# First layer of a fused attention and two-layer kernel in tiles of 256 and 384 tokens, and a shorter start

## The chip, the cores and the metric

The kernel runs on one core of a Trainium2 chip. The metric is the device time of one execution in microseconds. A core has five engines with an instruction queue each: TensorE (PE, matmuls; its weight loads are shown as PEld), VectorE (DVE), ScalarE (ACT), GpSimd (POOL) and SyncE (SP), which here only issues DMAs. They work on SBUF, and matmuls write the banks of PSUM; semaphores order them.

## The reference

Windowed attention over 4 x 576 tokens with 8 heads of 64, then two dense blocks on the 2304 x 512 result.

```python
# q, k, v: (4, 8, 576, 64)
rel = pos[:, None] - pos[None, :]
mask = (rel >= 0) & (rel < 64)
scores = np.where(mask, np.matmul(q, k.T) / 8, -1e9)      # k.T: last two axes
attn = np.exp(scores - scores.max(-1)); attn /= attn.sum(-1) + 1e-09
x = attn @ v                                   # to (2304, 512)
h = x @ moe_w_in;   g = s * max(h, 0)**2 + b;               x = g @ moe_w_out
h = x @ moe2_w_in;  g = max(h, 0) + alpha * min(h, 0);      out = g @ moe2_w_out
# w_in: (512, 2048), w_out: (2048, 512), s and b scalars, alpha: (2048,)
```

## The kernel before, in words

Every operand of the dense layers is split into a high part (rounded to fp32r) and a low part (the rest), and each product is three matmuls: high by high, high by low, low by high.

**Attention** goes in 18 groups of 128 tokens (`j`). For a group TensorE computes the scores (`scores`, L313, 64x128 blocks), VectorE adds the mask and takes the maxima (`maxima`, L498 to L507), ScalarE the exponents (`exponents`, L392, in two halves of four), VectorE divides by the sum (`normalise`, L518), TensorE transposes (L322), both copy (`copy_pt`, L400 and L524), TensorE multiplies by v (`values`, L334), and ScalarE and VectorE write the result as high and low part into `x` (`x_high` L406, `x_low` L530).

**A dense layer** is cut into tiles of 384 tokens, six per layer, and each tile into 16 steps, one for each 128 columns of the hidden width. Step `c` has an `up(c)`: 12 matmuls of 384 columns into the PSUM bank `hid[c % 2]` (L252), and a `down(c)` in two halves: in the first layer 12 matmuls of 384 columns into four accumulators `acc` (L291), in the second 9 of 512 columns into three (L297). Between them stands the chain of the step. First layer: relu on ScalarE (L367), times itself and s on VectorE (L474), high part with b added on ScalarE (L377), low part on VectorE (L488). Second layer: L479, L482, L380, L492.

**The order is written out by hand**, engine by engine, as one loop over steps. TensorE does `down(c)`, then `up(c + 2)`, so `up` is two steps ahead. In a step `s` ScalarE does relu and high part of `c = s + 1`, then what the attention has for it in this step (`copy_pt`, `x_high`), two weight splits in tile 0, and the exponents; VectorE does square and low part of `s + 1`, `copy_pt`, `x_low`, `normalise`, `maxima`. Behind all that, in the last step of a tile, both copy the accumulators out (`copy_out`, L426 and L548). The attention of the next tile's groups runs beside a tile: `group_at` gives the slot of a group, slots 5 steps apart, the first in the last step of the tile before; scores in step `slot`, the exponents' halves in `slot` and `slot + 1`, `normalise` in `slot + 2`, transposes in the middle of `down(slot + 3)`, values in the middle of `down(slot + 4)`.

**The start.** Groups 0, 1 and 2 are computed ahead of the loop; after each, `first_ups` does the part of `up(0)` and `up(1)` on its 128 tokens. Then come `scores(3)` and `up(2)`.

**Weights** arrive in pieces of 256 KB, four slots in SBUF, w_in and w_out in turn. GpSimd makes high and low part of the first 8 pieces; for the others ScalarE makes the high part (L387) and GpSimd the low part (L246), two pieces per step of tile 0. The second layer's are split in the first layer's last tile. The first layer's result goes through DRAM (`x2_scratch`) and comes back tile by tile.

Of the kernel before, what the change touches and what calls it, by code (L numbers as in the profile page):

```python
# [15 lines left out]
def build(nc, qk_in, v_in, w_in_a, w_out_a, w_in_b, w_out_b, consts_in, out):  # L16
# [6 lines left out]
    TILE = 384  # L23
    NO = TILE // 128
    NT = TOKENS // TILE
# [6 lines left out]
    assert TOKENS % TILE == 0 and NT % 2 == 0 and ND == PAIRS  # L32
# [6 lines left out]
    arrives = {piece: n + 1 for n, piece in enumerate(PIECES)}  # L39

    def slot_of(j):
        return NF * (j // NO - 1) + PITCH * (j % NO) - 1

    group_at = {slot_of(j): j for j in range(NO, NJ)}

    with ExitStack() as ctx:
# [8 lines left out]
        x = sb("x", [128, 2, 2, ND, TILE], F32R)  # L55
        g = sb("g", [128, 2, 2, TILE], F32R)
        relu = sb("relu", [128, 2, TILE])
        outs = sb("outs", [128, ND * TILE])
# [3 lines left out]
        x2_in = qk[:, 0:ND * TILE].rearrange("p (c t) -> p c t", c=ND)  # L62
# [19 lines left out]
        x2_dram = nc.dram_tensor("x2_scratch", (NT, 128, ND * TILE), F32, kind="Internal").ap()  # L82
# [12 lines left out]
        w_split = sem("w_split")  # L95
# [12 lines left out]
        last_copied = [sem(f"last_copied{a}") for a in range(NO)]  # L108
# [17 lines left out]
        def banks(j):  # L126

            return ((bank_x, bank_y), (acc[0], acc[1]), (acc[2], acc[3]))[j] if j < NO else (bank_x, bank_y)

        def x_at(j):  # L130
            return j // NO % 2, slice(j % NO * 128, (j % NO + 1) * 128)

# [9 lines left out]
        def _(sp):  # L142
            def load_piece(n):
                down, f = PIECES[n % NP]
                if n % NP >= SLOTS or n >= NP:
                    sp.wait_ge(w_split, n - SLOTS + 1)
                src = ((w_in_a, w_out_a), (w_in_b, w_out_b))[n // NP][down][f]
                sp.dma_start(piece[:, n % SLOTS, :], src).then_inc(piece_here[n // NP][n % SLOTS], 16)
# [11 lines left out]
            def store(dst, src, t):  # L160
                sp.wait_ge(acc_read_act, t + 1)
                sp.wait_ge(acc_read_dve, t + 1)
                sp.dma_start(dst, src).then_inc(stored, 16)

            def load_x2(t):
                sp.dma_start(qk[:, 0:ND * TILE], x2_dram[t - NT]).then_inc(x2_loaded, 16)

            load_qk(0)
            load_qk(1)
            load_v(0)  # L170
            load_piece(0)
# [8 lines left out]
            load_v(2)  # L180
            load_piece(6)
            load_piece(7)
            load_qk(3)
            for n in range(8, BY_POOL + SLOTS):
                load_piece(n)
            load_v(3)
            load_qk(4)
            load_v(4)
            for i in range(NF):
                for n in range(BY_POOL + SLOTS + 2 * i, min(BY_POOL + SLOTS + 2 * i + 2, NP)):  # L190
                    load_piece(n)
                if i == 1:
                    load_qk(5)
                if i == 5:
                    load_v(5)
                    load_qk(6)
            load_v(6)
            load_qk(7)
            load_v(7)
            for t in range(1, NT - 1):  # L200
                store(x2_dram[t - 1], outs[:, :], t - 1)
                for j in range(NO * t + 5, min(NO * t + 8, NJ)):
# [4 lines left out]
            store(x2_dram[NT - 2], outs[:, :], NT - 2)  # L207
            sp.wait_ge(s_done, NJ)
            sp.wait_ge(stored, 16)
            load_x2(NT)  # L210
            for n in range(NP + SLOTS, 2 * NP):
                load_piece(n)
            store(x2_dram[NT - 1], outs[:, :], NT - 1)
            out_v = out.rearrange("(t a p) d -> t p a d", p=128, a=NO)
            for t in range(NT, 2 * NT - 1):
                sp.wait_ge(x2_lo, ND * (t - NT + 1))
                sp.wait_ge(stored, 16 * (t - NT + 2))
                load_x2(t + 1)
                store(out_v[t - NT], outs[:, 0:NO * DM].rearrange("p (a d) -> p a d", a=NO), t)
            for a in range(NO):  # L220
# [442 lines left out]
```

## Time and profile before

| | |
|---|---|
| median of three runs | 910.15 us (909.05 to 910.41) |
| the profiled execution | 910.64 us, span 908.9 us |
| granted TensorE clock | 1.0 |
| TensorE busy, matmuls | 886.0 us (97%) |
| VectorE busy | 410.2 us (45%) |
| ScalarE busy | 285.9 us (31%) |
| GpSimd busy | 91.5 us (10%) |

All rows come from the profiled execution, whose own time is 1.7 us over its span. Busy times are sums over instructions; an engine can be busy 45% on average and still be late in one stage. In rows of the timeline the instructions of one line that follow on each other are merged, and the end of a matmul contains its way through the array, so the time of a block of matmuls is read from its start to the start of the next.

### The profile page before, as it was taken

How to read it: one execution, taken by the hardware profiler on the slowest of the kernel's cores; microseconds unless marked ns; L12 is line 12 of the kernel's file. 1: busy time of each engine (PE TensorE's matmuls, PEld its weight loads, DVE VectorE, ACT ScalarE, POOL GpSimd, SP SyncE). 2: the span in 40 equal slices, each digit the busy share in tenths (PEclk: the TensorE clock that was granted, in tenths of full speed). 3: DMA queues.
4: the chain of work that ended last, by engine and by line, in shares of the span. 5: the costliest groups of instructions: out<-in, count | busy, mean ns of one | idle time of the engine just before them, and what ended most of it. 6: DMA issues, size and time to landing. Idle time of an engine off the chain costs nothing.

```text
span 908.9 us, 13847 instructions
## 1 busy us (share of the span) xinstructions
PE 886.0 (97%) x5664; PEld 831.9 (92%) x5664; DVE 410.2 (45%) x945; ACT 285.9 (31%) x717; POOL 91.5 (10%) x81
## 2 busy tenths in 40 slices
PE   4799999999999999999999999999999999999998
PEld 4799999999999999999999999999999999999987
DVE  5155544444444444444354444454453444444443
ACT  4156543434434443444455211111121111111111
POOL 5135500000000000000356200000000000000000
PEclk9999999999999999999999999999999999999999
DMA  6425421102112110300344200200200200200000
GB/s 232 167 79 166 123 87 54 53 25 78 39 53 88 53 53 24 129 6 1 122 124 127 93 0 1 70 1 1 70 1 1 70 0 1 70 1 1 35 1 35
DMA packets 18767, 53.06 MB, mean 58 GB/s; under 512 B 2064, under 2 KB 2064, under 8 KB 18704
## 3 DMA queue, kind: packets, MB, share of 16 engines
q1 hardware_dynamic: 18704, 52.18, 17.5%
q8 instruction: 44, 0.72, 0.3%
q14 instruction: 19, 0.16, 0.1%
HBM read 42.74 MB, written 9.44 MB: 57 GB/s over the span
## 4 chain that ended last, share of the span: by engine, by line
PE 91%; ACT 4%; DVE 3%; DMA 1%; issue 1%; DVEq 0%
PE hid L252 44%; PE acc L297 22%; PE acc L291 20%; PE bank_x L334 2%; ACT p L392 2%; PE bank_x L313 1%; DMA qk<-in_qk 1%; PE bank_x L322 1%; PE bank_y L322 1%; DVE relu L474 1%; ACT g L377 1%; DVE g L488 1%; DVE p L518 1%; ACT relu L367 1%; PE acc L322 0%
## 5 line engine op out<-in xcount | busy, mean ns | idle before, releaser
L252 PE MATMUL hid<-x,w_in 128*128 128x384 f32 (+1 forms) x2352 | 447.8, 340 | 4.5 <-DVE x L530 4.5
L252 PEld LDWEIGHTS hid<-x,w_in 128*128 128x128 f32 x2352 | 418.1, 193 | 16.1 <-DVE x L530 5.1
L291 PE MATMUL acc<-g,w_out 128*128 128x384 f32 x1152 | 223.6, 337 | 2.7 <-ACT outs L426 2.7
L297 PE MATMUL acc<-w_out,g 128*128 128x512 f32 x864 | 215.4, 393 | 0.4 <-DVE g L492 0.4
L291 PEld LDWEIGHTS acc<-g,w_out 128*128 128x128 f32 x1152 | 199.8, 188 | 4.8 <-issue 3.8
L297 PEld LDWEIGHTS acc<-w_out,g 128*128 128x128 f32 x864 | 160.7, 188 | 30.0 <-DVE g L492 0.8
L380 ACT ACTIVATE g<-relu 128x384 fp32r<-128x384 f32 x96 | 50.4, 525 | 332.7 <-DVE relu L482 332.7
L474 DVE SCALAR_TENSOR_TENSOR relu<-relu,consts 128x384 f32<-128x384 f32 x96 | 71.0, 739 | 165.6 <-ACT relu L367 165.6
L479 DVE TENSOR_SCALAR relu<-hid,consts 128x384 f32<-128x384 f32 x96 | 59.3, 617 | 161.5 <-PE hid L252 161.5
L488 DVE SCALAR_TENSOR_TENSOR g<-relu,consts,g 128x384 fp32r<-128x384 f32 x96 | 59.9, 624 | 65.8 <-ACT g L377 65.8
L367 ACT ACTIVATE relu<-hid 128x384 f32<-128x384 f32 x96 | 46.8, 488 | 132.6 <-PE hid L252 132.6
L377 ACT ACTIVATE g<-relu,consts 128x384 fp32r<-128x384 f32 x96 | 59.2, 617 | 78.7 <-DVE relu L474 78.7
L492 DVE TENSOR_TENSOR g<-relu,g 128x384 fp32r<-128x384 f32 x96 | 53.6, 559 | 56.8 <-ACT g L380 56.8
L246 POOL TENSOR_TENSOR w_in<-piece,w_in 128x512 fp32r<-128x512 f32 x32 | 43.8, 1371 | 330.9 <-ACT w_in L387 330.5
L392 ACT ACTIVATE p<-p,negmx 128x128 f32<-128x128 f32 x144 | 56.0, 390 | 42.0 <-DVE negmx L507 42.0
L482 DVE SCALAR_TENSOR_TENSOR relu<-hid,relu 128x384 f32<-128x384 f32 x96 | 53.5, 557 | 3.3
L246 POOL TENSOR_TENSOR w_out<-piece,w_out 128x512 fp32r<-128x512 f32 x32 | 42.5, 1332 | 73.8 <-ACT w_out L387 73.5
L392 ACT ACTIVATION_READ_ACCUMULATOR p<-p,negmx 128x1 f32 x144 | 27.0, 187 | 0.0
L518 DVE TENSOR_TENSOR p<-p,rowrec 128x1024 f32<-128x1024 f32 x18 | 25.0, 1390 | 0.6
L313 PE MATMUL bank_x<-qk 64*64 64x128 f32 x256 | 19.3, 294 | 4.8 <-DMA qk<-in_qk 4.8
L507 DVE CUSTOM_DVE_ANT_0 p<-bank_x,mask 128x128 f32<-128x128 f32 x64 | 18.3, 286 | 11.7 <-DVE mask L498 6.5
L313 PEld LDWEIGHTS bank_x<-qk 64*64 64x64 f32 x256 | 15.2, 143 | 8.4 <-issue 8.3
(54 smaller groups left out, 314.6 us busy)
## 6 DMA issues: line engine op xcount, KB each, us to landing
qk<-in_qk SPq DMA_DIRECT2D x18, 640.0 KB, 5.0
v<-in_v SPq DMA_DIRECT2D x18, 512.0 KB, 3.6
x_scratch<-outs SPq DMA_DIRECT2D x6, 768.0 KB, 4.0
qk<-x_scratch SPq DMA_DIRECT2D x6, 768.0 KB, 5.7
piece<-in_w_in_a SPq DMA_DIRECT2D x16, 256.0 KB, 2.8
piece<-in_w_out_a SPq DMA_DIRECT2D x16, 256.0 KB, 3.0
piece<-in_w_in_b SPq DMA_DIRECT2D x16, 256.0 KB, 2.8
piece<-in_w_out_b SPq DMA_DIRECT2D x16, 256.0 KB, 2.6
```

What stands on the lines that cost most here:

```text
L246: pool.tensor_tensor(lo, piece[:, n % SLOTS, :], hi.bitcast(F32), ALU.subtract).then_inc(w_split, 1)
L252: mm = pe.matmul(hid[f % 2][:, at], w_in[:, wi, f, dc, :], x[:, par, xi, dc, at], start=(dc == 0 and n == 0), stop=(dc == ND - 1 and n == 2))
L291: mm = pe.matmul(acc[dc][:, 0:TILE], w_out[:, wi, f, dc * 128:(dc + 1) * 128], g[:, f % 2, gi, :], start=(f == 0 and n == 0), stop=(f == N ...
L297: mm = pe.matmul(acc[a][:, :], g[:, f % 2, gi, a * 128:(a + 1) * 128], w_out[:, wi, f, :], start=(f == 0 and n == 0), stop=(f == NF - 1 an ...
L367: act.activation(relu[:, c % 2, :], hid[c % 2][:, 0:TILE], ACT.Relu).then_inc(hid_read, 1)
L377: act.activation(g[:, c % 2, 0, :], relu[:, c % 2, :], ACT.Identity, bias=b_sb).then_inc(g_hi, 1)
L392: act.activation(p[:, j % 2, i, :], p[:, j % 2, i, :], ACT.Exp, bias=negmx[:, j % 2, i:i + 1], scale=-1.0, accum_out=rowsum[:, j % 2, i:i ...
L474: dve.scalar_tensor_tensor(out=relu[:, c % 2, :], in0=relu[:, c % 2, :], scalar=s_sb, in1=relu[:, c % 2, :], op0=ALU.mult, op1=ALU.mult).t ...
L479: dve.tensor_scalar(relu[:, c % 2, :], hid[c % 2][:, 0:TILE], 0.0, alpha[:, f:f + 1], ALU.min, ALU.mult).then_inc(negative, 1)
L482: dve.scalar_tensor_tensor(out=relu[:, c % 2, :], in0=hid[c % 2][:, 0:TILE], scalar=0.0, in1=relu[:, c % 2, :], op0=ALU.max, op1=ALU.add). ...
L488: dve.scalar_tensor_tensor(out=g[:, c % 2, 1, :], in0=relu[:, c % 2, :], scalar=b_sb, in1=g[:, c % 2, 0, :].bitcast(F32), op0=ALU.add, op1 ...
L492: dve.tensor_tensor(g[:, c % 2, 1, :], relu[:, c % 2, :], g[:, c % 2, 0, :].bitcast(F32), ALU.subtract).then_inc(g_ready, 1)
```

## The change

- The first layer has seven tiles instead of six: three of 256 tokens, then four of 384. The second keeps its six of 384. `widths` and `starts` hold this; `C_A` is the number of steps of the first layer (112), `C_END` that of all (208).
- Only groups 0 and 1 are computed ahead of the loop, and `first_ups` is gone: after them come `scores(2)` and whole `up(0)`, `up(1)`, `up(2)` of 256 columns. Groups 2 and 3 run beside tile 0, 4 and 5 beside tile 1, 6 to 8 beside tile 2, then three per tile.
- The low parts of the first layer's w_out pieces from piece 8 on are made by VectorE (`split_low`), those of w_in by GpSimd. `w_split` becomes two semaphores.
- `copy_out` stands right behind relu and high part, or square and low part, ahead of the attention work of the step; ScalarE copies banks 0 and 2, VectorE 1 and 3 (in the second layer 1), each copy signals on its own, and TensorE waits bank by bank (`acc_free`).
- SyncE's order of loads in the start is another; the scratch tensor is laid out by 128 columns of d_model, so rows of 1 KB or 1.5 KB are written and rows of 1.5 KB read, where they were 6 KB.

```diff
+    WIDE = 384
+    NB = WIDE // 128
+    widths = [256] * 3 + [WIDE] * ((TOKENS - 768) // WIDE) + [WIDE] * (TOKENS // WIDE)
+    starts = [sum(widths[:t]) % TOKENS for t in range(len(widths))]
+    NT = len(widths)
+    NA = NT - TOKENS // WIDE
+    C_A, C_END = NA * NF, NT * NF
+    EARLY = widths[0] // 128
...
+    def by_dve(n):
+        return BY_POOL <= n < NP and PIECES[n][0] == 1
...
     def slot_of(j):
-        return NF * (j // NO - 1) + PITCH * (j % NO) - 1
+        t = tile_of(j)
+        return NF * (t - 1) + PITCH * (j - starts[t] // 128) - 1
...
             load_qk(0)
             load_qk(1)
+            load_piece(0)
             load_v(0)
-            load_piece(0)
             load_piece(1)
             load_v(1)
             sp.dma_start(consts[:, :], consts_in).then_inc(consts_here, 16)
-            load_qk(2)
             load_piece(2)
             load_piece(3)
+            load_qk(2)
...
-            for j in range(NO):
+            for j in range(EARLY):
                 scores(j)
-            for j in range(NO):
+            for j in range(EARLY):
                 transposed(j)
                 values(j)
-                first_ups(j)
-            scores(NO)
-            up(LAG)
-            for c in range(2 * NT * NF):
+            scores(EARLY)
+            for c in range(LAG + 1):
+                up(c)
+            for c in range(C_END):
...
+            def acc_free(t, n):
+                if n % 2 == 0:
+                    pe.wait_ge(acc_read_act, 2 * (t - 1) + n // 2 + 1)
+                elif t <= NA:
+                    pe.wait_ge(acc_read_dve, 2 * (t - 1) + n // 2 + 1)
+                else:
+                    pe.wait_ge(acc_read_dve, 2 * NA + t - NA)
...
                     hi(c)
+                if i == NF - 1 and t >= 0:
+                    copy_out(t)
                 if s - 3 in group_at:
                     copy_pt(group_at[s - 3])
...
-                if i == NF - 1 and t >= 0:
-                    copy_out(t)
...
+            def split_low(n):
+                high, low = weights(n)
+                dve.wait_ge(piece_hi, n - BY_POOL + 1)
+                dve.tensor_tensor(low, piece[:, n % SLOTS, :], high.bitcast(F32),
+                                  ALU.subtract).then_inc(split_dve, 1)
...
+                if t == 0:
+                    for n in range(BY_POOL + 2 * i, min(BY_POOL + 2 * i + 2, NP)):
+                        if by_dve(n):
+                            split_low(n)
                 if s - 2 in group_at:
                     normalise(group_at[s - 2])
```

The rows below are the instructions in program order: line, operation, output and inputs, shape and count. On TensorE, the start before, from the scores of groups 1 and 2 to those of group 3 (L313 scores, L322 transposes, L334 values, L252 the parts of `up(0)` and `up(1)`):

```order
L313 MATMUL acc<-qk 64x128 x32
L322 MATMUL bank_x<-ident,p 128x128 x4
L322 MATMUL bank_y<-ident,p 128x128 x4
L334 MATMUL bank_x<-pt,v 64x64 x16
L252 MATMUL hid<-x,w_in 128x128 x24
L322 MATMUL acc<-ident,p 128x128 x8
L334 MATMUL acc<-pt,v 64x64 x16
L252 MATMUL hid<-x,w_in 128x128 x24
L322 MATMUL acc<-ident,p 128x128 x8
L334 MATMUL acc<-pt,v 64x64 x16
L252 MATMUL hid<-x,w_in 128x128 x24
L313 MATMUL bank_x<-qk 64x128
```

And now (L346 scores, L355 transposes, L367 values, L295 `up`, L320 `down`):

```order
L346 MATMUL acc<-qk 64x128 x16
L355 MATMUL bank_x<-ident,p 128x128 x4
L355 MATMUL bank_y<-ident,p 128x128 x4
L367 MATMUL bank_x<-pt,v 64x64 x16
L355 MATMUL acc<-ident,p 128x128 x8
L367 MATMUL acc<-pt,v 64x64 x16
L346 MATMUL bank_x<-qk 64x128
L346 MATMUL bank_y<-qk 64x128
...
L295 MATMUL hid<-x,w_in 128x256 x36
L320 MATMUL acc<-g,w_out 128x256 x24
```

One group's transposes and values and all 128-column matmuls on `hid` have left the start; 36 matmuls of 256 columns stand between `scores(2)` and the first `down`.

On VectorE, two steps of tile 0 with a group's second maxima (the last of them shown) and its `normalise`, before:

```order
L507 ISA p,negmx<-bank_y,mask 128x128
L507 ISA negmx 128x1
L474 SCALAR_TENSOR_TENSOR relu<-relu,consts 128x384
L488 SCALAR_TENSOR_TENSOR g<-relu,consts,g 128x384
L513 TENSOR_SCALAR rowsum<-rowsum 128x8
L515 RECIPROCAL rowrec<-rowsum 128x8
L518 TENSOR_TENSOR p<-p,rowrec 128x1024
```

And now:

```order
L539 ISA p,negmx<-bank_y,mask 128x128
L539 ISA negmx 128x1
L499 SCALAR_TENSOR_TENSOR relu<-relu,consts 128x256
L514 SCALAR_TENSOR_TENSOR g<-relu,consts,g 128x256
L524 TENSOR_TENSOR w_out<-piece,w_out 128x512
L545 TENSOR_SCALAR rowsum<-rowsum 128x8
L547 RECIPROCAL rowrec<-rowsum 128x8
L550 TENSOR_TENSOR p<-p,rowrec 128x1024
```

The low part of a w_out piece (L524) stands between the step's low part and `normalise`.

On ScalarE, the end of a tile whose last step has a group's scores (L367 relu, L377 high part, L392 exponents, L426 accumulators), before:

```order
L367 ACTIVATE relu<-hid 128x384
L377 ACTIVATE g<-relu,consts 128x384
L392 ACTIVATE p,rowsum<-p,negmx 128x128 x4
L426 ACTIVATE outs<-acc 128x384 x2
L367 ACTIVATE relu<-hid 128x384
```

And now:

```order
L401 ACTIVATE relu<-hid 128x256
L409 ACTIVATE g<-relu,consts 128x256
L455 ACTIVATE outs<-acc 128x256 x2
L424 ACTIVATE p,rowsum<-p,negmx 128x128 x4
L401 ACTIVATE relu<-hid 128x256
```

The two copies moved ahead of the exponents.

## Rows read from the trace of the kernel before

**Rows 1.** Waits of TensorE: line, released by, us in total, times, longest.

```profile
PE acc L313 <- DMA qk<-in_qk: 4.4, 1, 4.4
...
PE acc L291 <- ACT outs L426: 2.7, 4, 0.7
...
PE bank_x L322 <- DVE p L518: 0.3, 2, 0.2
```

**Rows 2.** Timeline of the start: start, duration (us), engine, line, operation; idle before.

```profile
11.28 1.97 DVE L518 TENSOR_TENSOR p<-p,rowrec 128x1024 f32<-128x1024 f32 x1
...
37.80 1.93 PE L322 MATMUL acc<-ident,p 128*128 128x128 f32 x8
...
39.76 0.60 ACT L400 ACTIVATE pt<-acc 128x512 f32<-128x512 f32 x1 [8.18 <-PE acc L322]
...
43.99 5.38 PE L252 MATMUL hid<-x,w_in 128*128 128x128 f32 x24 [1.41 <-DVE x L530]
...
51.22 4.11 PE L252 MATMUL hid<-x,w_in 128*128 128x384 f32 x12
55.16 4.33 PE L291 MATMUL acc<-g,w_out 128*128 128x384 f32 x24
```

**Rows 3.** TensorE at pace: timeline, and busy times by stretch (131.50:209.27 is one tile).

```profile
125.28 2.25 PE L291 MATMUL acc<-g,w_out 128*128 128x384 f32 x12
128.49 2.35 PE L252 MATMUL hid<-x,w_in 128*128 128x384 f32 x12
...
509.20 2.27 PE L252 MATMUL hid<-x,w_in 128*128 128x384 f32 x12
...
511.30 2.24 PE L297 MATMUL acc<-w_out,g 128*128 128x512 f32 x9
...
513.38 2.27 PE L252 MATMUL hid<-x,w_in 128*128 128x384 f32 x12
...
131.50:209.27 77.77, 77.10 (x600) 74.49 (x601) 34.93 (x103) 31.66 (x89) 0.00 (x0) 1.00 0.17 57
```

**Rows 4.** Timeline, ScalarE and VectorE: the chain of one step behind `up`.

```profile
121.31 0.49 ACT L367 ACTIVATE relu<-hid 128x384 f32<-128x384 f32 x1 [2.71 <-PE hid L252]
...
121.84 0.62 DVE L474 SCALAR_TENSOR_TENSOR relu<-relu,consts 128x384 f32<-128x384 f32 x1 [2.51 <-ACT relu L367]
...
122.49 0.62 ACT L377 ACTIVATE g<-relu,consts 128x384 fp32r<-128x384 f32 x1 [0.69 <-DVE relu L474]
...
123.14 0.62 DVE L488 SCALAR_TENSOR_TENSOR g<-relu,consts,g 128x384 fp32r<-128x384 f32 x1 [0.69 <-ACT g L377]
```

**Rows 5.** Timeline, ScalarE and VectorE: the steps of one group, at a tile's end.

```profile
128.96 0.40 ACT L392 ACTIVATE p<-p,negmx 128x128 f32<-128x128 f32 x1 [1.69 <-DVE negmx L507]
...
130.52 0.84 ACT L426 ACTIVATE outs<-acc 128x384 f32<-128x384 f32 x2
131.26 0.47 ACT L367 ACTIVATE relu<-hid 128x384 f32<-128x384 f32 x1
...
133.94 0.40 ACT L392 ACTIVATE p<-p,negmx 128x128 f32<-128x128 f32 x1 [0.89 <-DVE negmx L507]
...
135.94 0.49 ACT L367 ACTIVATE relu<-hid 128x384 f32<-128x384 f32 x1 [0.35 <-PE hid L252]
...
138.74 1.23 DVE L518 TENSOR_TENSOR p<-p,rowrec 128x1024 f32<-128x1024 f32 x1
```

**Rows 6.** Groups by line and shape, VectorE's copies: busy us, mean ns of one.

```profile
L548 DVE COPY outs<-acc 128x384 f32<-128x384 f32 x12 | 6.1, 549 | 0.0
...
L550 DVE COPY outs<-acc 128x512 f32<-128x512 f32 x5 | 3.4, 685 | 0.1
```

**Rows 7.** Timeline of tile 0: ScalarE's splits of a step, and a square on VectorE.

```profile
54.92 0.62 ACT L387 ACTIVATE w_out<-piece 128x512 fp32r<-128x512 f32 x1
...
55.97 0.39 ACT L392 ACTIVATE p<-p,negmx 128x128 f32<-128x128 f32 x1
...
62.17 1.63 DVE L474 SCALAR_TENSOR_TENSOR relu<-relu,consts 128x384 f32<-128x384 f32 x1
```

More of the change, by code:

```diff
@@ L38, in build, with tile_of @@
     NP = len(PIECES)
-    arrives = {piece: n + 1 for n, piece in enumerate(PIECES)}
+    place = {piece: n for n, piece in enumerate(PIECES)}
+    def by_dve(n):
+        return BY_POOL <= n < NP and PIECES[n][0] == 1
+    def tile_of(j):
+        return next(t for t in range(NA) if starts[t] <= j * 128 < starts[t] + widths[t])
     def slot_of(j):
-        return NF * (j // NO - 1) + PITCH * (j % NO) - 1
-    group_at = {slot_of(j): j for j in range(NO, NJ)}
+        t = tile_of(j)
+        return NF * (t - 1) + PITCH * (j - starts[t] // 128) - 1
+    group_at = {slot_of(j): j for j in range(EARLY, NJ)}
     with ExitStack() as ctx:
@@ L126, in banks, with split_count @@
         def banks(j):
-            return ((bank_x, bank_y), (acc[0], acc[1]), (acc[2], acc[3]))[j] if j < NO else (bank_x, bank_y)
+            return ((bank_x, bank_y), (acc[0], acc[1]))[j] if j < EARLY else (bank_x, bank_y)
         def x_at(j):
-            return j // NO % 2, slice(j % NO * 128, (j % NO + 1) * 128)
+            t = tile_of(j)
+            return t % 2, slice(j * 128 - starts[t], (j + 1) * 128 - starts[t])
+        def split_count(n):
+            same = sum(by_dve(m) == by_dve(n) for m in range(n + 1))
+            return (split_dve if by_dve(n) else split_pool), same
         block = ctx.enter_context(nc.Block())
@@ L192, in _ @@
                 if i == 1:
+                    load_qk(4)
+                if i == 4:
+                    load_v(4)
+                if i == 5:
                     load_qk(5)
-                if i == 5:
+                if i == 9:
                     load_v(5)
[L196 to L202, printed above, removed]
+            for t in range(1, NA - 1):
+                store(t - 1)
+                for j in range((starts[t + 1] + 256) // 128, min((starts[t + 1] + widths[t + 1] + 256) // 128, NJ)):
                     load_qk(j)
@@ L274, in up @@
+                if c >= 2:
+                    pe.wait_ge(hid_read, c - 1)
+                if t in (0, NA):
+                    pe.wait_ge(*split_count(NP * (t // NA) + place[0, f]))
+                if f == 0 and t < NA:
+                    pe.wait_ge(x_lo, (starts[t] + n_tok) // 128)
+                if f == 0 and t >= NA:
+                    pe.wait_ge(x2_lo, ND * (t - NA + 1))
                 for dc in range(ND):
-                    mm = up_part(t % 2, f, dc, slice(0, TILE))
+                    for n, (wi, xi) in enumerate(((0, 0), (0, 1), (1, 0))):
+                        mm = pe.matmul(hid[f % 2][:, 0:n_tok], w_in[:, wi, f, dc, :], x[:, t % 2, xi, dc, 0:n_tok],
+                                       start=(dc == 0 and n == 0), stop=(dc == ND - 1 and n == 2))
```

250 lines of the change are left out of this document (114 added, 136 removed).

## The prediction

> **What bounds the kernel now.** I read the waits of TensorE first. Outside the start it waits for almost nothing: the largest entry that belongs to the loop is 2.7 us in four waits for ScalarE's copy of the accumulators [rows 1]. So the loop runs at the pace of the matmuls, and only three things can move the time: when the loop starts, how many matmul nanoseconds it holds, and whether the other engines still keep up once a step is shorter.
>
> The timeline of the start shows the first. The first `down` begins at 55.16 [rows 2]. Ahead of it stand three groups' attention and three runs of 24 matmuls with 128 columns, each 5.38 us long, at about 220 ns a matmul; even after the last of them, which began at 43.99, the 12 matmuls of 384 columns that start at 51.22 take 3.94 us, 328 ns each. Only from 55.16 on are they at 174 to 180 ns (4.33 us for 24). The granted clock of the page is 1.0 in every slice, so that row doesn't show it; the durations say that TensorE ran at 1.2 GHz until 55.16 and at 2.4 GHz behind it; before it rose it had done 5.3 us of 128-column matmuls, scores, and 3.94 us of 384-column ones.
>
> The second comes from the steady state: 12 matmuls of 384 columns take 2.10 us (509.20 to 511.30; 2.08 in the first layer, 173.6 ns each), 9 of 512 take 2.08 (231 ns) [rows 3]. A tile of the first layer takes 77.77 us; 16 steps of 24 matmuls are 66.7 of it and one accumulator wait 0.7 [rows 1], which leaves 10.4, or **3.5 us per attention group**. Scores cost 3.21 - 2.08 = 1.13 us.
>
> The third is the chain behind each `up`: relu, square, high part, low part start 0.53, 0.65 and 0.65 us apart and the last takes 0.62 [rows 4]. It is done 2.65 us after the matmuls of `up` ended, and TensorE needs the result only two blocks, 4.17 us, later: 1.5 us to spare. In the steps of a group the exponents stand in ScalarE's queue, 1.56 us for a half (128.96 to 130.52) [rows 5]. The relu behind the second half still waited 0.35 us for TensorE, so it was just not late.
>
> **The change, term by term.** Times are of the profiled execution, 910.64 us (span 908.9), 0.5 above the median of 910.15.
>
> *Start.* The product p of group 0 is normalised at 13.25 [rows 2]; nothing waits for a third group's queries any more (the 4.4 us in [rows 1]), so its transposes start at 13.3. ScalarE copies them 1.96 later (39.76 against 37.80), at 15.3, then does the last half of group 1's exponents until 17.4. Normalising group 1 meets GpSimd's weight splits and takes 0.4 + 1.97: transposes of group 1 at 19.8. From transposes to the first matmul on x it is 6.19 us (37.80 to 43.99): 26.0. There `scores(2)` stands first, because it waits for x_lo of both groups, 1.95 us at half clock; `up(0)` at 27.9. 12 matmuls of 256 columns at half clock take 2.7 us; if the clock rises 3.94 us into them, as before, 18 are at half clock and 18 at 117.5 ns (below): **`down(0)` at 34.0 instead of 55.16: -21.1 us**. If the clock comes 3 us sooner or later, this moves by 1.5.
>
> *Matmuls of the loop.* Behind that point the first three tiles have 48 + 45 blocks of 12 instead of 32 + 29. A matmul of 256 columns isn't in the trace. From below: the line through 512 and 384 gives 114.6 ns, and the 128-column runs at half clock, halved, say that a weight load allows 108 to 112. From above: 384's cost less 128/2.4 is 120.3 (all of its surplus fixed), and 173.6 if the load of new weights set the pace of the 384-column stream. I take 117.5, between the two near rows. 93 x 12 x 0.1175 = 131.1 against 61 x 12 x 0.1736 = 127.1: **+4.0 us** (+0.8 to +7.2 between the near ends). The Trainium skill (TensorE: Matmul & The Clock Gate, Back-to-back issue gap) gives N/2.4 + 2.5 ns, an estimate of 109.2 here; for 384 columns it gives 162.5 where the trace has 173.6, so the trace doesn't agree. By that rule for both widths this term would be 2.9 us.
>
> *One more group in the loop* (group 2's transposes and values, group 3's scores): **+3.5 us**, from the same row as above.
>
> *Steps of 256 columns, tiles 1 and 2.* Copies lose 136 ns per 128 columns on VectorE [rows 6], ScalarE about 0.11; so relu to square is 0.42, then 0.52, 0.54, and low part 0.49. I lay one group out from the end of `up(s+1)`, a block being 1.41 us. `down(s)` to 1.41, scores to 2.54, exponents start 0.47 behind (128.49 to 128.96), at 3.01, and end at 4.57. Relu(s+2) at 4.57, its low part starts at 6.05. The second half's exponents start 0.87 behind the low part's start now (131.26 to 133.94 less 1.81), 0.74 with the narrower one: 6.79 to 8.35. Relu(s+3) is queued behind them, at 8.35 instead of 7.07. Its low part is ready at 10.35, and `down(s+3)`, due at 9.69, waits 0.7. The multiplication of `normalise` is queued behind that low part: it starts 0.97 behind its start now (135.94 to 138.74 less 1.83), 0.84 then, takes 1.23 and ends at 11.9; the transposes, half a block behind 10.4, i.e. at 11.1, wait 0.85. **1.55 us per group**, where groups in tiles of 384 have none. Groups 4 and 6 are scored at a tile's end, where VectorE now copies two banks before `maxima`: exponents 0.7 later, 2.25 each. Three at 1.55 and two at 2.25 make **+9.2 us**. A faster or slower matmul changes only the part of the five steps that isn't set by this chain, about half.
>
> *Tile 0.* ScalarE has two splits per step besides, 1.05 us (54.92 to 55.97 in [rows 7]); VectorE gets one low part of a w_out piece, about 0.6, right ahead of `normalise` and `maxima`; GpSimd keeps one of 1.3 us. Where an operation of VectorE with both inputs in SBUF falls on one of GpSimd's, it ends behind it: the square at 62.17 took 1.63 instead of 0.62, a normalisation 1.97 instead of 1.23. Laid out the same way, group 3 costs 1.5 (relu(s+3) at 9.3) and 2.2 (normalised at 14.2, transposes due at 12.0): 3.7. Group 2, whose exponents stand between relu(0) and relu(1) while TensorE already has three `up` behind it, costs 1.65 + 1.7 + 2.25 = 5.6. In plain steps ScalarE's own round (relu, wait for a square held up by GpSimd, high part, two splits) is 3.3 us against TensorE's 2.82: 0.5 in each of three steps. Sum 10.8; before, late normalisations made TensorE wait 0.3 [rows 1]. **+10.5 us**, 7 to 14. The rule of the Trainium skill on that port (SBUF — State Buffer, Who interferes with whom) is that whoever starts first holds it for the whole instruction and the other blocks fully; the trace agrees (0.62 against 1.63), and the rule speaks against giving VectorE a share of the splits, though GpSimd's share halves.
>
> *Accumulators.* The four waits go, **-2.7 us**: the copy of a bank now starts when `down` ends, and with 256 columns 0.4 us each hides behind `up`'s 1.4. The stores and x2 loads with shorter rows, and the other order of the weight and query loads, I count at nothing: a x2 load has over half a tile before its first use, and pieces are asked for two steps (6.6 us) ahead of their use. If the queries and values that stand between them in SyncE's queue hold them up, tile 0 gets 1 to 4 us longer; that is in its upper end.
>
> Sum: -21.1 + 4.0 + 3.5 + 9.2 + 10.5 - 2.7 = **+3.4 us**, span 912.3, 914.0 in a profiled execution, 913.5 against the median.
>
> **Rivals.**
> *Faster: the short steps hide their chains.* It decides at one place: the relu behind the second half of the exponents. If the chain of 256 columns is 0.7 us shorter than I make it, or exponents start earlier, relu(s+3) is in time, `down(s+3)` doesn't wait and the normalisation comes in time too. For it: before, the same place was met with 0.35 to spare, so two engines' overheads have been small. Against: the exponents (1.56 us a half) don't shrink with the tile, the steps do, by 1.35 us each. With half of the 20 us of waits gone the time is 903.5; with all gone 894.
> *Worse tile 0.* Pieces late, or TensorE, idle half the time in group 2's steps, back at 1.2 GHz for some microseconds: +4 to +8, 918 to 922. For it: four slots of pieces now turn over in 6.6 us instead of 8.3; against: in tile 0 before, the waits of TensorE name no piece [rows 1].
> *Weight loads set the pace at 256 columns.* With 145 ns a matmul, about +16 to +30 us, 930 to 943. Against: with the same load the 128-column runs took about 220 ns at half clock [rows 2], so 110 at full clock if the load goes with it.
>
> **How the numbers follow.** Forecast 55 (own range 909 to 918, of which 14 within the bound below), faster rival 27 (6 of it within), worse tile 0 12, weight loads 6. A measurement of this kernel tells 0.2%, 1.8 us, from no change: faster than 908.3, 0.21; within 0.20; slower than 912.0, 0.59. Range 904 to 921: it leaves out the deep end of the faster rival (8 in 100), the weight loads, and the far end of tile 0.
>
> **What would show it.** Right: `down(0)` near 34; 12 matmuls of 256 columns every 1.41 us; in each group of tiles 1 and 2 TensorE waits for g and then for p, 0.7 to 0.85 us each; tile 0 takes about 63 us from `down(0)` to tile 1, of which 11 are waits; tiles of 384 columns keep 77.1. The `acc` waits gone. Wrong: `up` blocks of over 1.5 us, no waits for g or p in tiles 1 and 2, or ScalarE waiting for pieces.

## The result, and the profile after

The change makes the kernel about 1% slower. The median is 918.94 us (918.77 to 920.44, 4 runs), against 910.25 for the kernel before on the same chip: a ratio of 1.0102 [1.0085, 1.012]. Forecast were 913.5, in a range of 904 to 921. The profiled execution took 918.83 (span 917.0) where the one before took 910.64 (span 908.9): +8.1 us of span to be explained, where the sum gave +3.4.

The waits of TensorE in the profile after (line, released by, us in total, times, longest):

```profile
PE bank_x L355 <- DVE p L550: 12.2, 8, 4.4
PE acc L320 <- DVE g L514: 8.3, 9, 2.5
PE bank_x L346 <- DMA qk<-in_qk: 4.8, 1, 4.8
```

Of [rows 1] the waits for ScalarE's copy of the accumulators are gone, as forecast. New are 8.3 us for g and 12.2 for p; 4.4 of the latter is the start's first group. So the kernel traded a late start for a loop in which VectorE's results are late. Cut into stretches, the span shows where (start:end, length, then the busy time of PE, PEld, DVE, ACT and POOL, the granted clock, the DMA share, GB/s). The stretches are from the first `down` to tile 1, tile 1, tile 2, the first layer's four wide tiles, and two pieces of tile 0:

```profile
33.08:100.27 67.19, 56.87 (x519) 54.44 (x517) 40.26 (x102) 35.93 (x97) 14.29 (x11) 0.92 0.37 115
100.27:156.62 56.35, 53.98 (x531) 51.95 (x530) 25.56 (x81) 23.41 (x71) 0.00 (x0) 1.00 0.16 53
156.62:219.35 62.73, 59.08 (x602) 56.14 (x601) 30.55 (x105) 27.88 (x89) 0.00 (x0) 1.00 0.20 67
219.35:515.20 295.85, 295.85 (x2153) 289.24 (x2153) 134.20 (x338) 130.38 (x331) 39.32 (x31) 1.00 0.22 69
37.20:39.92 2.72, 2.72 (x12) 2.72 (x13) 1.51 (x9) 2.27 (x10) 1.29 (x1) 0.50 0.29 96
68.70:74.30 5.60, 5.60 (x26) 5.60 (x27) 2.21 (x4) 2.14 (x4) 1.28 (x1) 0.50 0.22 57
```

And of the kernel before, its tile 0 and its last four tiles of the first layer, between the same events:

```profile
55.16:131.50 76.34, 75.35 (x589) 72.18 (x589) 42.81 (x102) 41.89 (x111) 33.39 (x24) 1.00 0.38 116
209.27:507.10 297.83, 296.50 (x2152) 289.36 (x2153) 134.42 (x338) 129.46 (x325) 40.77 (x32) 1.00 0.22 70
```

From these the ledger of the span: the first `down` starts at 33.08 instead of 55.16 [rows 2], -22.1. The first 768 tokens take 67.19 + 56.35 + 62.73 = 186.3 us instead of 76.34 + 77.77 = 154.1 [rows 3], +32.2. The four wide tiles take 2.0 less. The second layer takes 401.8 in both. Together +8.1. The columns say more than the lengths: in the wide tiles PE is busy for the whole stretch, in tile 0 for 56.87 of 67.19 us, and there the granted clock is 0.92, with two pieces at 0.50. The two pieces are the work that follows a wait in this part of TensorE's timeline (start, duration, line, operation; idle before):

```profile
27.71 5.53 PE L295 MATMUL hid<-x,w_in 128*128 128x256 f32 x36
...
33.08 1.61 PE L320 MATMUL acc<-g,w_out 128*128 128x256 f32 x12
37.20 2.93 PE L320 MATMUL acc<-g,w_out 128*128 128x256 f32 x12 [2.50 <-DVE g L514]
39.92 1.69 PE L295 MATMUL hid<-x,w_in 128*128 128x256 f32 x12
...
45.11 0.65 PE L355 MATMUL bank_x<-ident,p 128*128 128x128 f32 x4 [2.42 <-DVE p L550]
...
60.78 1.70 PE L320 MATMUL acc<-g,w_out 128*128 128x256 f32 x12 [1.30 <-DVE g L514]
...
65.31 0.98 PE L320 MATMUL acc<-g,w_out 128*128 128x256 f32 x6 [1.39 <-DVE g L514]
68.70 1.12 PE L355 MATMUL bank_x<-ident,p 128*128 128x128 f32 x4 [2.41 <-DVE p L550]
...
71.75 2.71 PE L295 MATMUL hid<-x,w_in 128*128 128x256 f32 x12
```

Rows of twelve matmuls that read 1.6 us at full clock read 2.71 and 2.93 after the waits of 2.50 us and of 1.30 + 1.39 + 2.41 us: TensorE is at 1.2 GHz there (granted clock 0.50). The wait of 2.42 alone at 45.11 was not followed by a slow stretch.

What is late in tile 0 stands in VectorE's and GpSimd's rows ahead of the transposes at 45.11:

```profile
41.18 0.48 DVE L514 SCALAR_TENSOR_TENSOR g<-relu,consts,g 128x256 fp32r<-128x256 f32 x1 [0.64 <-ACT g L409]
...
41.70 0.69 DVE L524 TENSOR_TENSOR w_out<-piece,w_out 128x512 fp32r<-128x512 f32 x1
...
42.27 1.26 POOL L278 TENSOR_TENSOR w_in<-piece,w_in 128x512 fp32r<-128x512 f32 x1 [3.24 <-ACT w_in L419]
42.31 1.25 DVE L545 TENSOR_SCALAR rowsum<-rowsum 128x8 f32<-128x8 f32 x1
...
43.83 1.22 DVE L550 TENSOR_TENSOR p<-p,rowrec 128x1024 f32<-128x1024 f32 x1
```

VectorE does its share of the weight splits (L524), during which GpSimd begins its own, and the tiny operation on 8 row sums that should follow takes 1.25 us; it ends with GpSimd's. The same operation takes 0.17 elsewhere (below). So the multiplication of `normalise` begins 2.2 us after the end of g's low part at 41.66, not 0.4. By the rule that the prediction weighed (Trainium skill, SBUF — State Buffer, Who interferes with whom), whoever issues first gets the ports that VectorE and GpSimd share for its whole instruction, and the other is blocked. The trace agrees, here even for an operation on 8 elements a partition (1.25 against 0.17).

### The profile page after: what moved, and what is told of

Same layout as the page of the kernel before. It is cut to its first block, busy times and chain, and to the rows that moved or that the text cites. A ratio compares the mean times of both kernels' runs of the same rounds, so it can differ in the third digit from the quotient of the medians.

```text
span 917.0 us, 14625 instructions
## 1 busy us (share of the span) xinstructions
PE 882.8 (96%) x6000; PEld 828.6 (90%) x6000; DVE 421.1 (46%) x992; ACT 293.4 (32%) x751; POOL 73.8 (8%) x68
## 4 chain that ended last, share of the span: by engine, by line
PE 87%; DVE 6%; ACT 5%; issue 1%; POOL 0%; DVEq 0%; ACTq 0%; POOLq 0%
PE hid L295 41%; PE acc L330 22%; PE acc L320 19%; ACT p L424 3%; PE bank_x L367 2%; DVE relu L499 1%; DVE p L550 1%; PE bank_x L346 1%; ACT g L409 1%; PE bank_x L355 1%; PE bank_y L355 1%; DVE g L514 1%; ACT relu L401 1%; DVE p L539 1%; DVE rowsum L545 0%
## 5 line engine op out<-in xcount | busy, mean ns | idle before, releaser
L295 PE MATMUL hid<-x,w_in 128*128 128x384 f32 (+1 forms) x2496 | 441.3, 325 | 0.0
L295 PEld LDWEIGHTS hid<-x,w_in 128*128 128x128 f32 x2496 | 412.8, 190 | 11.2 <-issue 2.9
L320 PE MATMUL acc<-g,w_out 128*128 128x384 f32 (+1 forms) x1344 | 231.8, 317 | 8.5 <-DVE g L514 8.3
L320 PEld LDWEIGHTS acc<-g,w_out 128*128 128x128 f32 x1344 | 208.3, 191 | 12.0 <-DVE g L514 10.9
L499 DVE SCALAR_TENSOR_TENSOR relu<-relu,consts 128x384 f32<-128x384 f32 (+1 forms) x112 | 71.5, 639 | 164.9 <-ACT relu L401 164.7
L514 DVE SCALAR_TENSOR_TENSOR g<-relu,consts,g 128x384 fp32r<-128x384 f32 (+1 forms) x112 | 63.3, 565 | 78.1 <-ACT g L409 78.1
L409 ACT ACTIVATE g<-relu,consts 128x384 fp32r<-128x384 f32 (+1 forms) x112 | 63.9, 571 | 99.6 <-DVE relu L499 95.3
L401 ACT ACTIVATE relu<-hid 128x384 f32<-128x384 f32 (+1 forms) x112 | 49.2, 439 | 125.9 <-PE hid L295 125.9
L278 POOL TENSOR_TENSOR w_out<-piece,w_out 128x512 fp32r<-128x512 f32 x19 | 25.6, 1348 | 24.8 <-ACT w_out L419 24.6
L346 PE MATMUL bank_x<-qk 64*64 64x128 f32 x272 | 20.4, 292 | 6.3 <-DMA qk<-in_qk 4.8
L346 PEld LDWEIGHTS bank_x<-qk 64*64 64x64 f32 x272 | 16.0, 143 | 9.4 <-issue 8.5
L355 PE MATMUL bank_x<-ident,p 128*128 128x128 f32 x68 | 11.6, 296 | 12.2 <-DVE p L550 12.2
```

Of the source, the lines that this page charges most:

```text
L278: pool.tensor_tensor(lo, piece[:, n % SLOTS, :], hi.bitcast(F32), ALU.subtract).then_inc(split_pool, 1)
L295: mm = pe.matmul(hid[f % 2][:, 0:n_tok], w_in[:, wi, f, dc, :], x[:, t % 2, xi, dc, 0:n_tok], start=(dc == 0 and n == 0), stop=(dc == ND - ...
L320: mm = pe.matmul(acc[dc][:, 0:n_tok], w_out[:, wi, f, dc * 128:(dc + 1) * 128], g[:, f % 2, gi, 0:n_tok], start=(f == 0 and n == 0), stop= ...
L401: act.activation(relu[:, c % 2, at], hid[c % 2][:, at], ACT.Relu).then_inc(hid_read, 1)
L409: act.activation(g[:, c % 2, 0, at], relu[:, c % 2, at], ACT.Identity, bias=b_sb).then_inc(g_hi, 1)
L499: dve.scalar_tensor_tensor(out=relu[:, c % 2, at], in0=relu[:, c % 2, at], scalar=s_sb, in1=relu[:, c % 2, at], op0=ALU.mult, op1=ALU.mult ...
```

## The experiments

All ratios are against the kernel before, timed on the same chip in the same rounds.

**1. The accumulators alone.** The kernel before, with the copies bank by bank, ahead of the attention work, and a wait for each bank:

```diff
-                act.wait_ge(down_done, (t + 1) * NF)
-                for n in range(2):
-                    ins = act.activation(outs[...], acc[n][:, 0:width], ACT.Copy)
-                ins.then_inc(acc_read_act, 1)
+                for n in (0, 2):
+                    act.wait_ge(down_done, (t + 1) * NF)
+                    act.activation(outs[...], acc[n][:, 0:width], ACT.Copy).then_inc(acc_read_act, 1)
...
+                        if f == 0 and t > 0:
+                            acc_free(t, dc)
```

> The kernel before with one part of the change alone: accumulators copied bank by bank ahead of the attention work, ScalarE banks 0 and 2, VectorE 1 and 3, TensorE waiting bank by bank. Theory (the four waits of TensorE for outs, 2.7 us, go and nothing comes in their place in tiles of 384): 2.4 to 2.8 us less than before, span 906.3. Rival (the copies now push the exponents back, and the relu behind them is late, 0.35 us was its margin): two waits for g at each tile's end, time within 1 us of before.

Measured: 906.41 us, 0.9963 [0.995, 0.9976], span 904.6. No wait names the copies any more. From the first `down` to the end the kernel is 2.9 us shorter, so this part of the change is worth its 2.7 us. The other 1.4 of the 4.3 us of span lies at the start, where the first `down` begins at 53.77 although nothing was changed there: 0.5 before the 12 matmuls of 384 columns (50.72 instead of 51.22), and 0.9 in them, which took 3.05 us instead of 3.94, because TensorE reached 2.4 GHz within them. The granted clock, which reads 1.0 throughout the start in the profile before, shows the rise in this one:

```profile
50.72 3.21 PE L252 MATMUL hid<-x,w_in 128*128 128x384 f32 x12
53.77 4.32 PE L297 MATMUL acc<-g,w_out 128*128 128x384 f32 x24
```

```profile
50.00:52.00 2.00, 2.00 (x20) 1.67 (x13) 0.93 (x9) 0.81 (x5) 0.00 (x0) 0.50 0.00 0
52.00:54.00 2.00, 2.00 (x12) 2.00 (x11) 0.62 (x1) 1.31 (x7) 0.00 (x0) 0.85 0.03 8
54.00:56.00 2.00, 2.00 (x13) 2.00 (x12) 1.45 (x9) 2.00 (x6) 0.88 (x1) 1.00 0.00 0
```

**2. Everything but the narrow tiles.** The kernel after with 384 tokens in every tile and three groups alone, whole `up`s kept:

```diff
-    widths = [256] * 3 + [WIDE] * ((TOKENS - 768) // WIDE) + [WIDE] * (TOKENS // WIDE)
+    widths = [WIDE] * (2 * TOKENS // WIDE)
```

> The changed kernel with tiles of 384 in both layers and three groups ahead of the loop, then scores(3) and whole up(0), up(1), up(2) of 384 columns; copies and splits as in the changed kernel. It asks what of the start's gain came from the parts of 128 columns and what from the third group, and what the narrow tiles cost. Theory: the parts of 128 columns at half clock (3 x 5.4 us) were most of the long start and can go without narrow tiles; down(0) starts near 40 to 42 instead of 55.2, the loop is as before less the 2.7 us of accumulator waits, span 891 to 895, that is 15 to 18 us under before and 23 to 26 under the changed kernel. Rival (the gain of the start needs the group to go as well; with three groups the attention chains of the start are the bound): down(0) later than 48, span above 900.

Measured: 908.13 us, 0.9982 [0.9972, 0.9991], span 906.4. The size was missed by more than 11 us: the first `down` came at 44.81 (10.3 earlier than before, as whole `up`s of 384 columns replace three runs of 128), but from the first `down` to the end it took 861.6 us instead of 853.7, which gave most of that back:

```profile
PE bank_x L355 <- DVE p L554: 5.4, 3, 2.0
...
PE acc L320 <- DVE g L518: 1.6, 2, 1.1
```

So even wide tiles wait for p here, and 50:60 and 81:93 ran at a granted clock of 0.88 and 0.86. What stands ahead of p in this loop, and didn't in the one before, is VectorE's share of the splits. Experiments 4 and 6 take it out.

**3. Shorter exponents.** The kernel after with one exponent instruction over four heads in each half of groups 2 to 8, with the maximum and the sum of one head, which leaves out part of the computation:

```diff
-                for i in range(4 * half, 4 * half + 4):
-                    act.wait_ge(max_done, HEADS * j + i + 1)
+                    act.wait_ge(max_done, HEADS * j + 4 * half + 4)
+                    ph = p[:, j % 2, 4 * half:4 * half + 4, :]
+                    act.activation(ph, ph, ACT.Exp, ...).then_inc(exp_done, 4)
```

> The changed kernel, but for groups 2 to 8 (those beside tiles of 256 tokens) the four exponents of a half are one instruction over 512 columns with one head's maximum and sum, so a half takes about 0.6 us of ScalarE instead of 1.56; this leaves out part of the computation. Theory (the waits in narrow tiles come from the exponents' time in ScalarE's queue, which doesn't shrink with the tile): relu(s+3) is in time; the waits for g (8.3 us) and for p in tiles 1 and 2 (3.0) nearly vanish, the ones in tile 0 halve; 8 to 12 us less than the changed kernel, span 905 to 909. Rival (VectorE's normalise, queued behind the low part, and its clash with GpSimd make the waits): the waits for p stay at 0.6 in tiles 1 and 2 and 2.4 in tile 0, less than 4 us gained.

Measured: 919.08 us, 1.0098 [1.0079, 1.0118]. The waits for p stay at 0.60 and 2.42 and nothing is gained, as the rival had it. Yet the test doesn't decide, for it hardly shortened what it was to shorten: the one instruction must wait for all four maxima, three of them 0.21 us apart behind the first, and takes 0.72 itself, so the half ended only about 0.2 us sooner than with four exponents (1.56). Experiment 7 puts the question again.

**4. All splits on GpSimd.**

```diff
-        return BY_POOL <= n < NP and PIECES[n][0] == 1
+        return False
```

> The changed kernel with all low parts of the weights on GpSimd again, none on VectorE. Theory (GpSimd's operations hold back VectorE's, so two of 1.3 us in a step of 2.88 us hurt more than VectorE's own 0.6): tile 0 gets 2 to 6 us longer, by squares of over 1 us in plain steps. Rival (the low part right ahead of maxima and normalise is what makes tile 0's waits long): tile 0 gets 1 to 3 us shorter.

Measured: 913.61 us, 1.0043 [1.0028, 1.0058], span 911.9: 5.1 us shorter than the kernel after. The theory that VectorE's share helps GpSimd keep up, and so pays, is refuted; the rival holds, with more than the 1 to 3 us that it was given. In tile 0 the two waits for p fall from 2.42 and 2.41 to 1.31 and 1.47. The operations that GpSimd holds up are still there, as before (a normalisation of 2.10 us, a square of 1.50), but VectorE does less in between. Both slow stretches are still there too: the clock is 0.50 in 37.27:40 and again behind the wait of 1.47 (64.77:67).

**5. TensorE kept awake.** 64 matmuls of 256 columns into the unread half of a bank, ahead of five waits of tile 0; nothing reads what they add:

```diff
+            def filler(n):
+                for _ in range(n):
+                    pe.matmul(acc[1][:, 256:512], w_in[:, 0, 0, 0, :], x[:, 0, 0, 0, 0:256], start=False, stop=False)
...
+    FILL_G = {1: 16, 6: 8, 7: 8}
+    FILL_T = {2: 16, 3: 16}
```

> The changed kernel with 64 extra matmuls of 256 columns that nothing reads, in columns 256 to 511 of an accumulator bank, in tile 0 ahead of its five long waits: 16 ahead of down(1), 8 each ahead of down(6) and down(7), 16 ahead of each of the transposes of groups 2 and 3. They take 1 to 1.9 us each and end before what TensorE waits for. Theory (TensorE falls to 1.2 GHz behind its idle stretches; of the two half-clock stretches of the changed kernel, 37.2 to 39.9 is covered by a wait of the same length, 68.7 to 74.3 is paid): no stretch at clock 0.5 in tile 0 behind 33, 2 to 3 us less, span 914 to 915. Rival (the chain of ScalarE and VectorE sets the time there too): within 1 us of the changed kernel, waits longer by what the matmuls get faster.

Measured: 916.75 us, 1.0071 [1.0056, 1.0086], span 915.0: 2.0 us less than after. The clock of tile 0 is now 1.00:

```profile
33.46:99.00 65.54, 61.57 (x589) 59.14 (x588) 40.56 (x103) 36.74 (x101) 14.37 (x11) 1.00 0.41 123
```

So the fall to 1.2 GHz costs the kernel after about 2 us net. In part the faster matmuls only wait again: ahead of the third `down` there is now a wait for g of 1.39 us that the kernel after doesn't have.

```profile
42.11 0.98 PE L329 MATMUL acc<-g,w_out 128*128 128x256 f32 x6 [1.39 <-DVE g L525]
```

**6. Wide tiles, all splits on GpSimd.** Experiment 2 with the edit of experiment 4.

> The kernel with three groups alone, whole ups and tiles of 384, now with all low parts of the weights on GpSimd as before. Theory (VectorE's split right ahead of normalise, and the row sums held up behind it by GpSimd, made the waits of 5.4 us for p and 1.6 us for g in tile 0): these shrink to the 0.2 to 0.9 us of the kernel before, and the half-clock stretches behind them go too: 5 to 7 us less, span 899 to 902, about 8 us under before. Rival (they come from the shorter start, in which pieces and exponents are late): at most 2 us less, waits for p over 3 us.

Measured: 899.03 us, 0.9881 [0.9864, 0.9897], span 897.1: 9.3 us under experiment 2, more than the 5 to 7 expected. Its waits:

```profile
PE acc L320 <- DVE g L518: 1.1, 1, 1.1
PE bank_x L355 <- DVE p L554: 1.0, 1, 1.0
```

The splits on VectorE were what ate experiment 2's gain, and the clock in the two stretches (0.88, 0.86) went with them: it is 1.00 in both here.

**7. A quarter of the exponents.** The kernel after with one exponent instead of four in each half of groups 2 to 8, which leaves out the rest, and with -30 for the mask's value, so that what is left stays finite:

```diff
-                for i in range(4 * half, 4 * half + 4):
+                for i in range(4 * half, 4 * half + (1 if few else 4)):
```

> The changed kernel, but for groups 2 to 8 only the first of the four exponents of a half is computed, waiting for its own maximum alone; the mask's value is -30 so that the rest stays finite. This leaves out part of the computation. A half now takes 0.5 us behind the first maximum instead of 1.56 (the 512-column instruction of the earlier try had to wait for all four maxima and ended only 0.25 us sooner, so it told nothing). Theory (the relu behind the second half is late by ScalarE's queue): in tiles 1 and 2 no waits for g (2.9 us) and p (3.0 us); in tile 0 the waits for g (5.4) shrink to under 2, those for p by about 1 us each; 7 to 11 us less in all. Rival (VectorE's queue makes them): the five waits for p of 0.6 stay.

Measured: 906.77 us, 0.9965 [0.9952, 0.9978], span 905.0: 12.0 us less than after. In tiles 1 and 2 a single wait of 0.38 us is left of ten; 56 us there have PE busy for 55.42:

```profile
99.90:155.90 56.00, 55.42 (x548) 53.80 (x546) 27.84 (x85) 19.68 (x47) 0.00 (x0) 1.00 0.16 53
```

In tile 0 the first wait for g fell from 2.50 to 0.96, but the waits for p stayed:

```profile
36.42 1.69 PE L320 MATMUL acc<-g,w_out 128*128 128x256 f32 x12 [0.96 <-DVE g L515]
...
43.26 0.66 PE L355 MATMUL bank_x<-ident,p 128*128 128x128 f32 x4 [2.42 <-DVE p L551]
```

**8. The splits moved, not removed.** The kernel after with VectorE's split behind `normalise` and `maxima` of its step instead of ahead:

```diff
-                if t == 0:
-                    for n in range(BY_POOL + 2 * i, min(BY_POOL + 2 * i + 2, NP)):
-                        if by_dve(n):
-                            split_low(n)
...
                 if s - 1 in group_at:
                     maxima(group_at[s - 1], 1)
+                if t == 0:
+                    for n in range(BY_POOL + 2 * i, min(BY_POOL + 2 * i + 2, NP)):
+                        if by_dve(n):
+                            split_low(n)
```

> The changed kernel with VectorE's low part of a w_out piece behind normalise and maxima in its step instead of ahead of them. Theory (the place is what hurts: 0.6 us ahead of normalise and then row sums that wait 1.1 us for GpSimd): as with all splits on GpSimd, 4 to 6 us less, waits for p in tile 0 near 1.4 instead of 2.4. Rival (the work itself on VectorE hurts wherever it stands, since it then delays the square of the next step): within 1.5 us of the changed kernel.

Measured: 912.31 us, 1.0024 [1.0014, 1.0033], span 910.5: 6.5 us less than after, a little more than expected and 1.4 more than taking the splits off VectorE altogether. VectorE's with one of GpSimd's, and then TensorE's rows:

```profile
41.16 0.17 DVE L545 TENSOR_SCALAR rowsum<-rowsum 128x8 f32<-128x8 f32 x1
...
41.60 1.23 DVE L550 TENSOR_TENSOR p<-p,rowrec 128x1024 f32<-128x1024 f32 x1
...
41.85 2.11 POOL L278 TENSOR_TENSOR w_in<-piece,w_in 128x512 fp32r<-128x512 f32 x1 [2.70 <-ACT w_in L419]
...
42.74 1.76 DVE L524 TENSOR_TENSOR w_out<-piece,w_out 128x512 fp32r<-128x512 f32 x1
```

```profile
37.33 2.93 PE L320 MATMUL acc<-g,w_out 128*128 128x256 f32 x12 [2.50 <-DVE g L514]
...
42.88 0.66 PE L355 MATMUL bank_x<-ident,p 128*128 128x128 f32 x4 [0.40 <-DVE p L550]
...
63.48 0.66 PE L355 MATMUL bank_x<-ident,p 128*128 128x128 f32 x4 [0.60 <-DVE p L550]
...
65.12 1.59 PE L295 MATMUL hid<-x,w_in 128*128 128x256 f32 x12
```

The row sums take 0.17, GpSimd's own operation is held up (2.11 instead of 1.26), because `normalise` began before it, and then VectorE's split (1.76), for which TensorE doesn't wait. The waits for p are 0.40 and 0.60. The first wait for g is still 2.50. At 65.12 twelve matmuls take 1.59 us: the second slow stretch is gone, where it was still there in experiment 4.

Experiments 7 and 8 are a crossed pair. With a quarter of the exponents the waits for g shrink and those for p in tile 0 stay; with the split out of the way those for p in tile 0 shrink, and the waits for g are 7.3 us in all, where they were 8.3. In tile 0 the two kinds of wait have two causes; in tiles 1 and 2, where nothing is split, those for p go with the exponents too.

**9. The start put in order too.** Experiment 6, and in the start ScalarE does group 1's second exponents, and VectorE group 1's normalisation, ahead of the copies of group 0:

```diff
             exponents(1, 0)
-            copy_pt(0)
             exponents(1, 1)
+            copy_pt(0)
             x_high(0)
...
             normalise(0)
+            normalise(1)
             copy_pt(0)
```

> The kernel with three groups alone, whole ups, tiles of 384 and all low parts on GpSimd, with two moves in the start: ScalarE does the second half of group 1's exponents ahead of its copy for group 0 (it stood idle 4.6 us there), VectorE normalises group 1 right behind group 0. Theory (TensorE's 4.1 us wait for group 1's p is a matter of that order): p of group 1 is ready near 15, its transposes start near 18.5 instead of 22.5, group 2's follow 3 to 4.5 us sooner, and down(0) starts at 40.5 to 41.7 instead of 44.7; 3 to 4 us less, span 893 to 894. Rival (maxima of group 2 or the clock then set the start): under 1.5 us.

Measured: 895.5 us, 0.9846 [0.983, 0.9862], span 893.8. It beats both kernels, 1.5% under the one before. The first `down` comes 4.5 us sooner than in experiment 6 (44.72); the span is 3.3 shorter:

```profile
40.26 2.25 PE L320 MATMUL acc<-g,w_out 128*128 128x384 f32 x12
```

**10. The same help for the narrow tiles.** The kernel after with the edits of experiments 4 and 9, so that it differs from experiment 9 in the widths and the number of early groups alone (with the order of the loads that goes with them).

> The changed kernel (three narrow tiles, two groups alone) with the two things that the other runs found: all low parts on GpSimd, and the same two moves in the start. Theory: down(0) starts 1.5 to 3 us sooner (its transposes of group 1 waited 1.8 us for p, and then its copy), the loop is as with GpSimd's splits; span 909 to 910.5, and the three narrow tiles still lose some 15 us to tiles of 384 with three groups alone. Rival (with its faults mended the two-group start pays): span under 900.

Measured: 912.02 us (909.46 to 913.6, 10 runs), 1.0015 [1.0005, 1.0025], span 909.3. Its first `down` is at 30.61, 9.65 earlier than in experiment 9, and yet it ends 15.5 us later: between the first `down` and the end the narrow tiles, with the third group moved into the loop, cost 25.2 us. That is the price of the idea itself, and the head start that it buys is 9.65.

## Why the prediction was right, and where it wasn't

The forecast case came true: slower, by the mechanism that it gave. The size was short by 4.7 us of span. By its own steps:

- **Start.** -22.1 for a forecast of -21.1. The transposes of group 1 stood at 19.47 (19.8 forecast), `up(0)` at 27.71 (27.9). Right; the 36 matmuls behind it took 5.37 us where 6.1 were laid out, so fewer of them ran at half clock.
- **Matmuls of the loop.** The term was mis-sized. In experiment 7, in a stretch where nothing is waited for, blocks of twelve follow each other every 1.44 us, 120.0 ns a matmul:

```profile
95.20 1.60 PE L320 MATMUL acc<-g,w_out 128*128 128x256 f32 x12
96.64 1.60 PE L295 MATMUL hid<-x,w_in 128*128 128x256 f32 x12
98.08 1.60 PE L320 MATMUL acc<-g,w_out 128*128 128x256 f32 x12
```

  That is the upper of the two near bounds, 120.3: all of the surplus of 384 columns is fixed per matmul. The term is then 93 x 12 x 0.120 - 127.1 = +6.8 instead of +4.0. The lower near bound was worked out wrongly: the line through 231 and 173.6 ns gives 116.2 for 256 columns, not 114.6; the value taken, 117.5, was near that end. The estimate from the Trainium skill (TensorE: Matmul & The Clock Gate, Back-to-back issue gap), 109.2, is off by 10.8 ns; the page gives that formula for an isolated matmul, not for a stream of weight loads and matmuls such as this one. The rival in which weight loads set the pace at 145 ns is out.
- **Steps of 256 columns, tiles 1 and 2.** Right in kind. In each group TensorE waits first for g, then for p (forecast 0.7 and 0.85):

```profile
107.17 0.98 PE L320 MATMUL acc<-g,w_out 128*128 128x256 f32 x6 [0.66 <-DVE g L514]
108.75 0.66 PE L355 MATMUL bank_x<-ident,p 128*128 128x128 f32 x4 [0.60 <-DVE p L550]
```

  On ScalarE the relu follows the exponents with no idle time between, where [rows 5] had 0.35; this was the place at which the faster rival would have been decided:

```profile
104.73 0.39 ACT L424 ACTIVATE p<-p,negmx 128x128 f32<-128x128 f32 x1
...
105.12 0.36 ACT L401 ACTIVATE relu<-hid 128x256 f32<-128x256 f32 x1
```

  TensorE is idle for 2.4 us of tile 1 and 3.7 of tile 2 (length less busy time, above): 6 us for a forecast of 9.2. The groups at a tile's end were put at 2.25 each, but the waits for g are 0.44 to 0.67 in all five and those for p 0.60. The copies of two banks ahead of `maxima` cost less than I laid out.
- **Tile 0.** This step failed: +10.5 was forecast, the rows show 14.0. TensorE is idle for 10.3 us, which is the sum as forecast; the 1.3 lost in the first slow stretch (12 matmuls in 2.72 instead of 1.44) and the 2.4 in the second (5.60 where the same work takes 3.2 in experiment 8) were not in it. The fall to 1.2 GHz stood in the rival "worse tile 0", at 12 in 100, instead of in the forecast. It happened, behind the waits of group 2 and again of group 3. Its net price is 2 us (experiment 5), not 4 to 8: in the first of the two stretches the faster matmuls of experiment 5 only wait 1.39 us for g afterwards. The idle time was right partly by luck: the waits for p are 2.42 and 2.41 for a forecast of 2.25 and 2.2, but I had them from a normalisation held up by GpSimd (1.97), and in fact it took 1.22 and the row sums ahead of it 1.25.
- **One more group, 3.5.** Not measured by itself. With the terms above, the first three tiles come to 6.8 + 3.5 + 6 + 14 = 30.3, against a measured 33.8: 32.2 of ledger, 1.3 for two accumulator waits that are gone, and 0.3 for waits for p that tile 0 had before. Of the 3.5 that are left, restarts explain some: behind a wait twelve matmuls take 0.1 us longer (60.78 to 62.31 is 1.53, not 1.44), and there are 16 waits in these tiles. The rest has no place that I can show.
- **Accumulators.** -2.7 forecast; the four waits are gone. Two of them lay in the first 768 tokens and two in the stretch of the wide tiles (1.3 us, all that TensorE was idle there), which is 2.0 shorter. Experiment 1 shows the part by itself, 2.9 us from the first `down` on.
- **Queues and loads at nothing.** Right for the loop: no wait of TensorE in it names a piece, a query or a store, ScalarE waits for no piece, and the second layer is unchanged at 401.8. The order of the loads and the shorter rows were not run by themselves.

Part of the errors cancelled: the start came 0.9 us sooner than forecast, the waits of tiles 1 and 2 were put 3.2 too high and the gain of the accumulators 0.6 too low; against that stand 2.8 of the matmuls, 3.2 of tile 0 (0.3 of its waits was there before) and the 3.5 left over.

What the sum did not see is that two parts of the change work against each other: VectorE's share of the splits was costed only as 0.6 us in two steps. By experiment 6 the new start with whole `up`s, the copies and the order of the loads together were worth 11.8 us of span without the narrow tiles, and VectorE's share of the splits costs 9.3 of that with wide tiles and 5.1 with narrow ones.

## What to carry to other kernels

When a step gets shorter, list what in it does not shrink: here 1.56 us of exponents in ScalarE's queue, ahead of a relu with 0.35 us to spare, set the bound of steps that lost 1.35 us; moving VectorE's split out of the way left 7.3 of the 8.3 us of waits for g. When work is moved to an engine that looks half idle, ask what is queued behind it there and whose result that is: the same split cost 6.5 us more ahead of a normalisation than behind it. And a change of several parts should be run in parts: this one, slower by 8 us, contained one that is 11.8 us faster than the kernel it replaced (experiment 6), and with another order in the start it is 15 us faster (experiment 9).

## What the runs showed of the hardware that was not expected

- A VectorE operation on 128x8 elements took 1.25 us next to a GpSimd operation of 1.26, and 0.17 without. How small the operation is doesn't protect it. It goes both ways: a GpSimd operation that began 0.25 us after VectorE's normalisation took 2.11 (experiment 8).
- The granted clock fell to 0.50 (1.2 GHz) behind a wait of 2.50 us in tile 0 and behind three waits of 1.30, 1.39 and 2.41 us, but not behind one of 2.42 at 45.11. With waits of 0.48, 0.83 and 0.60 in the same place (experiment 8) it stayed at 2.4 GHz. The length of a wait alone doesn't decide: in experiment 10 the clock stayed at 1.00 behind the same wait of 2.50 us, and fell behind waits of 0.91 and 1.46. What decides it is open here.

```profile
34.71 1.69 PE L320 MATMUL acc<-g,w_out 128*128 128x256 f32 x12 [2.50 <-DVE g L514]
...
38.74 0.98 PE L320 MATMUL acc<-g,w_out 128*128 128x256 f32 x6 [0.91 <-DVE g L514]
...
41.19 1.12 PE L355 MATMUL bank_x<-ident,p 128*128 128x128 f32 x4 [1.46 <-DVE p L550]
```

- At 1.2 GHz twelve matmuls of 256 columns take 2.72 us, 227 ns each, less than twice the 120.0 at 2.4 GHz, so not all of a matmul's time goes by the clock.
- The moment at which the clock first rises differs between two executions whose starts hold the same work: 0.9 us of experiment 1's 4.3 us of span came from that alone.
